# Two changes to a fused attention and feed-forward kernel: pooled results upsampled by products on TensorE, and three sums of results moved to GpSimd

## The reference

```
q, k, v: (4, 8, 576, 64)                    batch, heads, sequence, head size
q_d, k_d, v_d = means over groups of 4 positions          (144 positions)
out_up    = repeat(softmax(q_d k_d^T / 8) v_d, 4)          pooled attention
out_local = softmax(q k^T / 8, masked to |i - j| < 4) v    banded attention
x = (out_up + out_local), as (2304 tokens, 512 features)
x = silu_1(x @ moe_w_in) @ moe_w_out        512 -> 2048 -> 512, silu(h)
x = silu_2(x @ moe2_w_in) @ moe2_w_out      the same, h * sigmoid(1.702 h)
```

## Time and profile before

| what | value |
| --- | --- |
| time, median of 3 runs | 809.66 us (809.51 to 809.9) |
| the profiled execution, its own time | 809.12 us |
| its span, first to last instruction | 807.3 us |
| TensorE busy | 789.9 us, 98% of the span |
| VectorE busy | 649.1 us, 80% |
| ScalarE busy | 530.7 us, 66% |
| GpSimd busy | 196.0 us, 24% |
| granted TensorE clock, mean | 1.00 |
| chain that ended last, by engine | PE 78%, POOL 8%, DVE 7%, issue 4% |

### The profile page before, as it was taken

One profiled execution on the slowest core, in us unless ns is written; L12 is line 12 of the kernel. 1 busy time (PEld: TensorE's weight loads), 2 busy tenths in 40 slices (PEclk: granted clock), 3 DMA queues, 4 the chain that ended last, 5 costly groups with the idle time before them and its releaser, 6 DMA issues.

```text
span 807.3 us, 15757 instructions
## 1 busy us (share of the span) xinstructions
PE 789.9 (98%) x5864; PEld 763.4 (95%) x5864; DVE 649.1 (80%) x911; ACT 530.7 (66%) x849; POOL 196.0 (24%) x197
## 2 busy tenths in 40 slices
PE   9888799999999999999999999999999999999998
PEld 5666599999999999999999999999999999999998
DVE  7999899999998778999678898899565688456466
ACT  5878865677655677565687556678455786465673
POOL 5889987520144320246100000000000000000000
PEclk9999999999999999999999999999999999999999
DMA  8777647887777887588877778868887777877773
GB/s 286 260 245 244 194 150 261 274 285 233 251 263 244 279 301 256 197 286 255 288 267 249 239 252 256 263 220 274 300 283 259 275 247 264 300 252 269 267 258 134
DMA packets 100763, 205.51 MB, mean 255 GB/s; under 512 B 8784, under 2 KB 56400, under 8 KB 100688
## 3 DMA queue, kind: packets, MB, share of 16 engines
q1 hardware_dynamic: 100688, 204.51, 76.0%
HBM read 160.96 MB, written 43.52 MB: 253 GB/s over the span
## 4 chain that ended last, share of the span: by engine, by line
PE 78%; POOL 8%; DVE 7%; issue 4%; DMA 1%; ACT 1%; SPq 0%; POOLq 0%; DVEq 0%; ACTq 0%
PE hid L330 41%; PE yp L356 35%; DVE gr L547 2%; POOL vpair L1015 2%; DVE wh L302 2%; POOL vavg L1019 1%; POOL pband L1009 1%; PE yp L372 1%; POOL G L1039 1%; POOL G L1040 1%; DVE xs L257 1%; DMA wr<-sums_out 1%; POOL G L1045 1%; POOL G L1043 1%; POOL x L271 0%
## 5 line engine op out<-in xcount | busy, mean ns | idle before, releaser
L330 PE MATMUL hid<-xs,wh 128*128 128x384 f32 x2016 | 351.2, 334 | 1.3 <-DVE hw L516 0.9
L330 PEld LDWEIGHTS hid<-xs,wh 128*128 128x128 f32 x2016 | 349.3, 188 | 2.3 <-issue 2.0
L356 PE MATMUL yp<-gr,wh 128*128 128x384 f32 x1968 | 342.4, 334 | 0.0
L356 PEld LDWEIGHTS yp<-gr,wh 128*128 128x128 f32 x1968 | 341.1, 188 | 0.3 <-issue 0.3
L293 ACT ACTIVATE wh<-wr 128x1024 fp32r<-128x1024 f32 (+1 forms) x164 | 164.6, 1004 | 151.3 <-PE hid L330 119.0
L547 DVE TENSOR_TENSOR gr<-G,gr 128x768 fp32r<-128x768 f32 x144 | 138.2, 967 | 52.6 <-ACT gr L428 52.6
L428 ACT ACTIVATE gr<-G 128x768 fp32r<-128x768 f32 x144 | 121.9, 846 | 67.3 <-PE yp L356 67.3
L302 DVE TENSOR_TENSOR wh<-wr,wh 128x1024 fp32r<-128x1024 f32 x76 | 91.5, 1203 | 16.5 <-ACT wh L293 16.4
L391 ACT ACTIVATE G<-G 128x1152 f32<-128x1152 f32 x48 | 55.8, 1162 | 0.0
L511 DVE TENSOR_TENSOR hv<-p,hid 128x384 f32<-128x384 f32 x48 | 26.4, 549 | 30.6 <-PE hid L330 26.5
L537 DVE TENSOR_TENSOR G<-hv,hid 128x384 f32<-128x384 f32 x48 | 26.4, 550 | 27.0 <-PE hid L330 26.9
(11 more groups left out here) (98 smaller groups left out, 762.6 us busy)
## 6 DMA issues: line engine op xcount, KB each, us to landing
wh<-rests SPq DMA_DIRECT2D x72, 512.0 KB, 3.7
wr<-sums_out SPq DMA_DIRECT2D x48, 512.0 KB, 4.8
wr<-in_w_out SPq DMA_DIRECT2D x36, 512.0 KB, 5.4
rests<-wh SPq DMA_DIRECT2D x36, 512.0 KB, 3.4
wr<-sums_in SPq DMA_DIRECT2D x40, 384.0 KB, 4.0
wr<-in_w_in SPq DMA_DIRECT2D x40, 256.0 KB, 3.6
qk<-in_qkT SPq DMA_DIRECT2D x11, 576.0 KB, 5.0
G<-in_w_in SPq DMA_DIRECT2D x12, 512.0 KB, 5.1
```

Source lines behind the costliest of these rows:

```text
L330: last = eng.matmul(hid[:, at, 0:HALF], lhsT=wh[:, w % SLOTS, part, a % 4, cc * P:(cc + 1) * P], rhs=xs[:, rest, q, cc, :], start=start an ...
L356: last = eng.matmul(yp[:, at + m, 0:HALF], lhsT=wh[:, w % SLOTS, part, p % 4, m * P:(m + 1) * P], rhs=gr[:, p, rest, :], start=start and p ...
```

## The change

Three parts of the attention loop and one of the layers are edited.

- `avg_product` no longer writes 144 columns beside the banded result. It reads each pooled probability column four times (`broadcast_to([P, SD // 2, FACTOR])`) and adds onto the 576 columns that `band_product` wrote (`start=False`), by 8 matmuls of 288 columns, each in a bank of its own half. The division by 4 moves into ScalarE's copy to `pta`, which is now written head by head.
- The finished 576 columns are copied to `x`: in iterations 3, 5, 7, 9, 11, 13, 15 and 16 (`TAKEN`) by VectorE, in the others by ScalarE at the place of the old scaled copy. `oavg` and VectorE's sum at L1176 are gone.
- TensorE transposes groups 0 to 3 right after `band_scores(u)`, and so ahead of `avg_scores(u)`; ScalarE copies all four ahead of the exponential at L1071. The banded tiles are cut differently (56, 58, ..., 57, 57, 58 queries), so that the halves of 288 columns match the banks.
- For blocks 0 and 1 the three sums at L565, L566 and L568 are made by GpSimd (`add_results`), after its four sums for the weight pairs 8 and 16 and ahead of those for pairs 9 and 17. The counts of `y_sum` follow, with a semaphore `y_add` for GpSimd's sums.

```diff
+        def add_results(eng, n, done, count):
+            eng.wait_ge(self.y_sum, results_of(n) + 1)
+            eng.tensor_tensor(quarter(n, 0, 1), yt[:, 0], yt[:, 2], ALU.add).then_inc(done, 1)
+            eng.tensor_tensor(yt[:, 1], yt[:, 0], yt[:, 1], ALU.add).then_inc(done, 1)
+            eng.wait_ge(done, count + 2)
+            eng.tensor_tensor(quarter(n, 1, 1), yt[:, 1], yt[:, 3], ALU.add).then_inc(done, 1)
...
                 add_bank(n, yt[:, 0], 2)
-                eng.wait_ge(self.y_sum, 5 * n + 1)
-                eng.tensor_tensor(quarter(n, 0, 1), yt[:, 0], yt[:, 2], ALU.add).then_inc(self.y_sum, 1)
-                eng.tensor_tensor(yt[:, 1], yt[:, 0], yt[:, 1], ALU.add).then_inc(self.y_sum, 1)
-                eng.wait_ge(self.y_sum, 5 * n + 3)
-                eng.tensor_tensor(quarter(n, 1, 1), yt[:, 1], yt[:, 3], ALU.add).then_inc(self.y_sum, 1)
+                if n not in ADDED:
+                    add_results(eng, n, self.y_sum, results_of(n) + 1)
...
@@ GpSimd, after the sums of pair q @@
+                if q % 8 == 0 and q // 8 - 1 in ADDED:
+                    n = q // 8 - 1
+                    eng.wait_ge(self.y_copy, 5 * n + 5)
+                    add_results(eng, n, self.y_add, 3 * ADDED.index(n))
...
-    nq = [FIRST_Q] + [NQ] * (NT - 1)
+    nq = [NQ - 2] + 6 * [NQ] + 2 * [NQ - 1] + [NQ]
+    TAKEN = (3, 5, 7, 9, 11, 13, 15, 16)
...
@@ ScalarE @@
-                    eng.activation(pta[:, j - NLG, :], src[:, 0:NA * AR], ACT.Copy).then_inc(p_cp, 1)
+                    eng.activation(pta[:, j - NLG].rearrange("p h c q -> p c h q"), by_head(src), ACT.Copy,
+                                   scale=1.0 / FACTOR).then_inc(p_cp, 1)
...
                 if not first:
-                    for j in range(NLG):
+                    for j in range(NG):
                         group(old, j)
...
-                if not first:
-                    for j in range(NLG, NG):
-                        group(old, j)
...
-                if not first:
+                if not first and u.n not in TAKEN:
                     eng.wait_ge(avg_out, old.n + 1)
-                    eng.wait_ge(x_done, 1 + old.n)
-                    eng.activation(oavg, po[:, OA:OA + SD], ACT.Copy,
-                                   scale=1.0 / FACTOR).then_inc(oavg_cp, 1)
+                    eng.activation(results(old), po[:, PO:PO + S], ACT.Copy).then_inc(x_done, 1)
...
@@ VectorE @@
-                if not first:
+                if u.n in TAKEN:
                     old = u.before()
-                    eng.wait_ge(oavg_cp, 1 + old.n + 1)
-                    eng.wait_ge(band_out, old.n + 1)
-                    eng.tensor_tensor(dst.rearrange("p (s r) -> p s r", r=FACTOR),
-                                      po[:, PO:PO + S].rearrange("p (s r) -> p s r", r=FACTOR),
-                                      oavg.unsqueeze(2).broadcast_to([P, SD, FACTOR]),
-                                      ALU.add).then_inc(x_done, 1)
+                    eng.wait_ge(avg_out, old.n + 1)
+                    eng.tensor_copy(results(old), po[:, PO:PO + S]).then_inc(x_done, 1)
...
@@ TensorE, avg_product @@
-                for h in range(2):
-                    for j in range(2):
-                        last = eng.matmul(po[h * D:(h + 1) * D, OA:OA + SD], lhsT=vavg[u.odd][:, j, h * D:(h + 1) * D],
-                                          rhs=pta[:, j, :].rearrange("p (c q) -> p c q", c=NA)[:, :, h * QT:h * QT + AQ],
-                                          start=(j == 0), stop=(j == 1))
+                for j in range(2):
+                    for half in range(2):
+                        for h in range(2):
+                            rhs = pta[:, j, h].rearrange("p c q -> p (c q)")[:, half * SD // 2:(half + 1) * SD // 2]
+                            last = eng.matmul(po[h * D:(h + 1) * D, PO + half * S // 2:PO + (half + 1) * S // 2],
+                                              lhsT=vavg[u.odd][:, j, h * D:(h + 1) * D],
+                                              rhs=rhs.unsqueeze(2).broadcast_to([P, SD // 2, FACTOR]),
+                                              start=False, stop=j == 1, skip_group_check=True)
...
```

More of the change, by code:

```diff
@@ L107, in __init__ @@
         self.bank, self.y_last = sem("bank"), sem("y_last")
+        self.y_add = sem("y_add")
     def first_raw(self, eng, p):
@@ L238, in features, with results_of, added @@
             return quarter(n, half, late)
+        ADDED = (0, 1)
+        def results_of(n):
+            return sum(2 if m in ADDED else 5 for m in range(n))
+        def added(eng, n):
+            eng.wait_ge(self.y_add, 3 * sum(m in ADDED for m in range(n)))
         def pair_out(eng, q):
@@ L251, in round_x @@
             if n >= self.BLOCKS:
-                eng.wait_ge(self.y_sum, 5 * (n - self.BLOCKS + 1))
+                eng.wait_ge(self.y_sum, results_of(n - self.BLOCKS + 1))
+                added(eng, n - self.BLOCKS + 1)
             eng.activation(xs[:, 0, q], features(n, q), ACT.Copy).then_inc(self.x_hi, 1)
@@ L339, in second @@
                 if i == 0:
-                    eng.wait_ge(self.y_sum, 5 * n)
+                    eng.wait_ge(self.y_sum, results_of(n))
                 elif i > 1:
@@ L434, in copy_out @@
                 if i == 0 and n:
-                    eng.wait_ge(self.y_sum, 5 * n)
+                    eng.wait_ge(self.y_sum, results_of(n))
+                    added(eng, n)
                 if i == 0 and n == 0:
@@ L736, in batch @@
                 if k == 1 and n:
-                    store(n - 1, 1, 0, (self.y_sum, 5 * n))
+                    store(n - 1, 1, 0, (self.y_sum, results_of(n)))
                 if k == 24:
@@ L744, in sync @@
                     n = w // BATCHES
-                    store(n, 0, 1, (self.y_sum, 5 * n + 2))
-                    store(n, 1, 1, (self.y_sum, 5 * n + 4))
+                    store(n, 0, 1, (self.y_sum, results_of(n) + 2))
+                    store(n, 1, 1, (self.y_sum, results_of(n) + 4))
             for m in range(2):
@@ L781, in build @@
     NQ = WIN - 2 * (FACTOR - 1)
-    FIRST_Q = S - (NT - 1) * NQ
-    q0 = [max(0, FIRST_Q + NQ * (t - 1)) for t in range(NT)]
-    nq = [FIRST_Q] + [NQ] * (NT - 1)
+    nq = [NQ - 2] + 6 * [NQ] + 2 * [NQ - 1] + [NQ]
+    q0 = [sum(nq[:t]) for t in range(NT)]
     starts = [min(max(q - (FACTOR - 1), 0), S - WIN) for q in q0]
@@ L817, in build @@
     assert DM == 512 and QT == D == P // 2 and starts[1] > 0 and q0[-1] - starts[-1] == 2 * (FACTOR - 1)
+    assert sum(nq) == S and q0[HALF] == S // 2
     assert all(a + WIN >= min(q + n + FACTOR - 1, S) for a, q, n in zip(starts, q0, nq))
@@ L867, in build @@
             sma = sb("sma", [AR, NA, 2])
-            spare = ffn.spare(HALF * P + SD)
-            ptb, oavg = spare[:, 0:HALF * P].rearrange("p (t n) -> p t n", t=HALF), spare[:, HALF * P:]
-            pta = sb("pta", [P, 2, NA * AR])
+            ptb = ffn.spare(HALF * P).rearrange("p (t n) -> p t n", t=HALF)
+            pta = sb("pta", [P, 2, 2, NA, AQ])
             sc = ps("sc", [P, 2, 512])
@@ L881, in build @@
             PO = 512 - q0[HALF]
-            OA = 832
         zero = sem("zero")
@@ L902, in build, with results @@
         band_out, avg_out = sem("band_out"), sem("avg_out")
-        oavg_cp, x_done = sem("oavg_cp"), sem("x_done")
+        x_done = sem("x_done")
         ffn.programs(keep, lambda name, shape: whole.enter_context(nc.psum_tensor(name, shape, F32)))
         block = whole.enter_context(nc.Block())
+        def results(u):
+            at = (2 * (u.half % 2) + u.odd) * T + (u.half // 2) * S
+            return x[:].rearrange("p c n -> p (c n)")[:, bass.ds(at, S)]
         def iterations(eng, start, body):
@@ L1061, in group, with by_head @@
                 else:
-                    eng.activation(pta[:, j - NLG, :], src[:, 0:NA * AR], ACT.Copy).then_inc(p_cp, 1)
+                    eng.activation(pta[:, j - NLG].rearrange("p h c q -> p c h q"), by_head(src), ACT.Copy,
+                                   scale=1.0 / FACTOR).then_inc(p_cp, 1)
+            def by_head(src):
+                from_h = src[:, 0:NA * AR].rearrange("p (c q) -> p c q", c=NA)
+                return bass.AP(from_h.tensor, from_h.offset, [from_h.ap[0], [AR, NA], [QT, 2], [1, AQ]])
             def body(u, first, last):
@@ L1123, in _ @@
             eng.sem_inc(p_cp, 3)
-            eng.sem_inc(oavg_cp, 1)
             iterations(eng, lambda u: None, body)
@@ L1168, in body @@
                     eng.reciprocal(rca[:], rca[:]).then_inc(a_rcp, 1)
-                if not first:
+                if u.n in TAKEN:
                     old = u.before()
-                    eng.wait_ge(oavg_cp, 1 + old.n + 1)
-                    eng.wait_ge(band_out, old.n + 1)
-                    at = (2 * (old.half % 2) + old.odd) * T + (old.half // 2) * S
-                    dst = x[:].rearrange("p c n -> p (c n)")[:, bass.ds(at, S)]
```

(11 more changed lines are left out.)

## The result

The changed kernel takes 820.9 us (median of 4 runs, 820.29 to 821.43) against 809.75; the ratio is 1.014, 95% interval 1.0127 to 1.0152. The profiled execution takes 820.62 us, its span is 818.8.

A forecast was written before the change was run, and what follows sets the result against it. TensorE was to become the bound of the attention loop: 10.1 of added work, 3.0 of late normalisation and -0.9 at the border make +12.2 on 809.12, 821.3; with 0.5 to the median, 821.8 us, range 816.5 to 827.

The forecast's parts named there:

- avg_product, start to next start: Attention loop, TensorE: eight pairs for four make avg_product 2.13 us, 1.48 us more each time, 23.7 us over 16.
- a turn of pure TensorE: Attention loop: an iteration of TensorE's work without waits becomes 6.57 us, over the present 6.03.
- work added less waits used up: Attention loop, TensorE: 23.7 us added, 13.7 absorbed by existing waits, 0.1 of new waiting in iteration 1: 10.1 us.
- late normalisation, six times: Attention loop: groups 2 and 3 wait for ScalarE's normalisation after iterations 4, 6, 8, 10, 12 and 14: 3.0 us.
- the layers: Border of blocks 0 and 1: three sums on GpSimd free VectorE, so TensorE's gap before `hw` goes: -0.9 us.
- the third rival: Attention loop: avg_product at 1.1 us or less, VectorE and GpSimd set the ring again, about 807.8 us; chance 0.05.
- the second's 1.4: avg_product: gaps stay at 0.15 us whatever the columns, group 1.4 us, turn 5.8, about 811 us; chance 0.1.
- the fifth: avg_product: heads no longer overlap in the new order, eight more gaps of 0.25 us, +32, 853 us; chance 0.03.
- The fourth: Attention loop: late normalisation in each even iteration, fed back through ScalarE, +1 us in seven, 826 to 829; chance 0.12.
- the sixth: Layers: GpSimd holds the pair's store and TensorE waits for weights at one border, +2, 824 us; chance 0.04.
- The rival with gaps that hardly grow: avg_product: gaps stay at 0.15 us whatever the columns, group 1.4 us, about 811 us; chance 0.1.
- VectorE's relief: Attention loop: VectorE loses L1176 (0.74 us) for a copy every second iteration; worth nothing, since TensorE sets the turn.

The follow-up runs named there:

- twice 288 columns: Changed kernel with every matmul of avg_product made twice at half the scale, 16 of 288 columns: 850.49 us, ratio 1.05 to the kernel before.
- 72 columns: Changed kernel with avg_product's 8 matmuls over 72 columns each, not repeated four times: 816.75 us against 809.75 for the kernel before.
- the fastest kernel: Changed kernel with both engines' old order, bf16 operands in avg_product, sums on GpSimd for block 0 only: 806.37 us against 809.52 for the kernel before.

## Why the prediction was right, and where its parts were off

The forecast was 821.8 us and the time is 820.9. Step by step, in us of span:

| step | predicted | measured |
| --- | --- | --- |
| avg_product, start to next start | 2.13 | 2.09 |
| a turn of pure TensorE | 6.57 | 6.53 |
| work added less waits used up (late normalisation apart) | +10.1 | +9.4 |
| late normalisation, six times (measured: all waits of these turns) | +3.0 | +2.8 |
| the layers | -0.9 | -0.86 |

The measured +9.4 is iteration 1, 8.41 - 6.92, iterations 2 to 15, 94.20 - 84.43, less the 2.8, and iteration 16, 7.57 - 6.60. The 2.8 is what the odd iterations from 5 on (but for 3) have over 6.53: 0.34, 0.34, 0.72, 0.45, 0.49, 0.46. Another 0.13 us come from the start, where iteration 1 begins at 9.00 for 8.87. Of the 0.7 us between 10.1 and 9.4, sixteen products at 2.09 for 2.13 are 0.6. The last step of the sum, 0.5 us from the profiled execution to the median, came out at 0.3. Two small slips in the working: the waits of iteration 16 are 0.67 us by the sum given there, not 0.5 (0.57 with the 3.23 that its products take in the trace), and the third rival's 807.8 lacks the 0.5 to the median.

The other rivals fell as well. The group of 2.16 us is far from the second's 1.4 and the third's 1.1, and its pairs at 0.24 leave no room for the fifth. The fourth would have added 1 us in each of seven turns; the waits came in six, 2.8 us in all. For the sixth, the first stage of the layers waits 0.3 us in all, for `hw` and not for weights.

**The price of columns.** The rival with gaps that hardly grow had a group of 1.4 us; the runs with 72, 288 and twice 288 columns settle it for the streaming. The page "TensorE: Matmul & The Clock Gate" of the Trainium skill, section Back-to-back issue gap, gives 81 ns at 128 columns and 131 at 512; by an estimate from it 288 columns would cost some 1.2 times what 144 do. These f32 pairs took 0.24 against 0.13 to 0.145. The measurement decides.

**The order.** I treated it as late normalisations on top of TensorE's turn. That gave nearly the right sum, since in this kernel a turn is the longest of three: TensorE's 6.53, the ring's 6.00 (6.87 with a rest of x in it, 7.1 to 7.3 with the rest of the weights), or ScalarE's chain behind the product, 6.81 to 7.02 where it has a rounding to do. But it hid how the loss is shared. The order alone costs 7.4 us, the products without it 8.9 (TensorE's order put back, with the gain of the sums in it), and together they cost 11.2. Either alone would explain most of the loss, and taking the products' cost away in the new order gives back only 3.4 us (7.7 with bf16 operands for 11.2). Part of this is the clock: the 7.4 and the 7.7 hold 2.6 and 2.7 us of loss by half clock, by their profiles, which the changed kernel doesn't pay. All 13 executions of the three kernels that keep the new order and leave TensorE room (order alone, bf16, 72 columns) have a mean granted clock of 0.989 to 0.996; all 28 of the seven that keep the product's full f32 columns have 0.999 or 1.000. So the ring itself is worth about 5 us. I had no term for the clock, and the forecast needed none only because TensorE stayed busy.

**Which engine is late.** The 2.8 for 3.0 is closer than its parts. The waits after iterations 4, 6 and 8 are 1.40 us for the predicted 1.2, those after 10, 12 and 14 are 1.40 for some 1.8: two misses that offset. For the turn after 8 I had GpSimd at nothing; 0.35 us of its wait is for GpSimd's normalisation, which VectorE's rest of the weights had made late. I gave the waits after iterations 10, 12 and 14 to ScalarE's rounding. That holds after 12, where the 0.49 stays without VectorE's rest. After 10 and 14 VectorE was the later one: without its rest 0.45 and 0.46 fall to 0.28 each, which is ScalarE's.

**The sums.** Right in size and mechanism at block 0, as the runs with and without them show: the gap comes and goes with them. GpSimd's 7.8 us lie in the predicted 5 to 9, though the first of the three took 3.29 for at most 3. The contention was dearer for VectorE than I took it, up to 2.86 us for an instruction of 1.21 at the next border, where it opened a gap of 0.26 that I had not forecast.

**VectorE's relief.** That losing L1176 is worth nothing under a bound of TensorE fits the turns of 6.53 with no idle on TensorE. With that bound and the ring away, iterations 2 to 8 take 5.5 us on average for 5.8 before. That this is VectorE's relief is argued and not shown: no run takes L1176 away alone, and this one also changes ScalarE's copies and the operands.

## What to carry to other kernels

Work moved to a fuller engine first fills that engine's waits (some 13.6 of the 23 us here), and is paid in full once its own turn is longer than the ring of waits; add its work start to start, without the waits, and compare with the present turn. A reorder inside a software pipeline can close a ring across iterations: follow the chain from the moved instruction until it meets itself, and take the turn as the longest of all rings, not their sum. When two changes set two such bounds, undoing one shows little. And look at the granted clock of every run that you compare: a run that gives TensorE room can lose part of its gain to a lower clock, as three did here.

## What was not expected of the hardware

In the profile of the run with the sums of block 0 on GpSimd TensorE stood idle for 1.88 us between two transposes of one group, which wait for nothing that the profile shows, and the granted clock then went from 1.00 to 0.50, that is from 2.4 to 1.2 GHz. Timeline, and windows of 2 us (after the busy times: clock, DMA share, GB/s):

```profile
31.42 0.33 PE L1228 MATMUL pt<-ident,pband 128*128 128x128 f32 x1 [1.88 <-issue]
...
34.60 1.24 PE L1308 MATMUL po<-pta,vavg 128*64 128x144 f32 x8
```

```profile
30.00:32.00 2.00, 0.58 (x7) 0.46 (x9) 0.83 (x1) 0.27 (x2) 1.84 (x3) 1.00 0.91 269
...
34.00:36.00 2.00, 2.00 (x37) 1.40 (x30) 1.97 (x4) 1.39 (x8) 0.79 (x1) 0.50 0.12 17
```

At the lower level avg_product took 1.24 us for 0.72. That turn lasted 8.3 us for 5.6. What held the issue isn't settled, and it isn't needed for the lower clock. The profiles hold nine more such stretches: a second one in this run, two each in the runs with the order alone, bf16 operands and 72 columns, and one each in the sums alone for both blocks and in the fastest kernel. Ahead of each of them TensorE had waited 1.35 to 1.71 us for GpSimd's normalisation of the banded probabilities. The turns last up to 8.42 us. The kernel before has three such waits, of 1.47 and 1.48 us, in its profile and kept full clock through them, and the run with 72 columns kept it in iteration 15 after the same 1.41 us as the run with the order alone, so the wait alone doesn't decide. None of the seven kernels with the product's full f32 columns shows such a stretch.

The kernels that leave TensorE room also spread more, 805.18 to 810.5 us for the fastest one against 820.29 to 821.43 for the changed one. The clock is at most part of the reason: the executions at 805.18 and 806.23 us had a mean of 0.997 and 1.000, the one at 810.5 had 0.994.
